# Batch 1's layer-norm statistics in one block, a pair earlier, and other work moved between engines in an attention, channel-mixer and gated-mixer kernel on one core

## What is computed

```
bits(q) == bits(k)                       # 6 hash bits by proj, bucket mask
attn = softmax(where(mask, q k^T / 8, -1e9)) v        -> x [2, 768, 512]
u    = x + real(fft(fft(x, tokens), features))
un   = (u - mean(u)) / sqrt(var(u) + 1e-6)
x2   = u + relu(un @ w_ch1) @ w_ch2                    # 512 -> 2048 -> 512
h    = gelu(x2 @ w_in);  U, v = split(h)
v_s  = w_sg @ (layernorm(v) * g_ln) + b_sg             # mixes tokens
out  = x2 + (U * v_s) @ w_out
```

## Time and profile before

| what | value |
|---|---|
| median of 3 runs | 735.77 us (735.25 to 736.75) |
| the profiled execution | 736.75 us, span of its instructions 734.9 us |
| PE busy | 716.1 us, 97% of the span, 3905 matmuls |
| DVE / ACT / POOL busy | 480.1 / 382.5 / 347.0 us |
| granted PE clock | 0.995 of full, mean |
| attention, transforms (about) | 0 to 260, 260 to 302.5 us |
| pairs 0 to 7, pairs 8 to 15 | 302.5 to 426.9, 426.9 to 558 us |
| gated mixer | from 563 us on |

### The profile page before, as it was taken

One profiled execution on the slowest core, in us unless ns is written; L12 is line 12 of the kernel. 1 busy time (PEld: TensorE's weight loads), 2 busy tenths in 40 slices (PEclk: granted clock), 3 DMA queues, 4 the chain that ended last, 5 costly groups with the idle time before them and its releaser, 6 DMA issues.

```text
span 734.9 us, 11758 instructions
## 1 busy us (share of the span) xinstructions
PE 716.1 (97%) x3905; PEld 590.5 (80%) x3905; DVE 480.1 (65%) x701; ACT 382.5 (52%) x708; POOL 347.0 (47%) x341
## 2 busy tenths in 40 slices
PE   8999999999999999999999999999999979999998
PEld 8857666666666899988888888999998868888886
DVE  6877787778786799876555677444434873247532
ACT  4867887888784635554444535445542553025300
POOL 4178878877887910224533261546542452004500
PEclk9999999999999999999999999999999989999999
DMA  4333323333243230121111212711003000010001
GB/s 97 69 73 67 77 60 71 73 67 70 60 101 115 69 113 1 42 74 58 58 58 58 70 46 101 243 58 58 29 1 144 0 1 0 29 58 1 0 15 72
DMA packets 71076, 45.20 MB, mean 62 GB/s; under 512 B 44996, under 2 KB 61560, under 8 KB 70520
## 3 DMA queue, kind: packets, MB, share of 16 engines
q1 hardware_dynamic: 70456, 41.19, 20.6%
q0 software_dynamic: 576, 3.43, 1.3%
HBM read 35.42 MB, written 3.15 MB: 52 GB/s over the span
## 4 chain that ended last, share of the span: by engine, by line
PE 86%; DVE 8%; ACT 2%; issue 2%; POOL 1%; DMA 1%; SPq 0%; POOLq 0%; ACTq 0%; DVEq 0%
PE PS L809 81%; DVE un L2007 2%; DVE mneg L1769 1%; PE PS L833 1%; PE PS L1096 1%; PE PS L1267 1%; PE PS L1313 1%; DMA ops<-mrow 1%; PE PS L1258 1%; PE PS L948 1%; DVE st L1995 0%; DVE W1L L2040 0%; DVE ops L1740 0%; DVE ops L1761 0%; DVE hL L2056 0%
## 5 line engine op out<-in xcount | busy, mean ns | idle before, releaser
L809 PE MATMUL PS<-ops 98*128 98x384 f32 (+1 forms) x576 | 134.8, 359 | 3.4 <-DMA ops<-mrow 1.1
L809 PEld LDWEIGHTS PS<-ops 98*128 98x128 f32 (+1 forms) x576 | 95.2, 189 | 44.1 <-ACT E L1380 19.6
L1769 DVE TENSOR_REDUCE mneg<-PS 128x1 f32<-128x768 f32 x96 | 91.5, 956 | 37.1 <-PE PS L809 36.5
L1380 ACT ACTIVATE E<-PS 128x384 f32<-128x384 f32 x192 | 83.5, 486 | 44.6 <-PE PS L809 43.8
L659 POOL TENSOR_TENSOR esum<-esum,E 128x768 f32<-128x768 f32 x56 | 102.5, 1830 | 2.9 <-ACT E L1380 0.3
L644 POOL TENSOR_TENSOR W2L<-W2R,W2H 128x1024 fp32r<-128x1024 f32 x16 | 38.5, 2407 | 114.7 <-ACT W2H L1364 114.7
L809 PE MATMUL PS<-BH,W1H 128*128 128x384 f32 x228 | 76.8, 337 | 2.8 <-DVE hL L2056 1.5
L2056 DVE SCALAR_TENSOR_TENSOR hL<-pre,hH 128x384 fp32r<-128x384 f32 x42 | 44.4, 1056 | 51.0 <-ACT hH L1625 51.0
L809 PE MATMUL PS<-BH,W1L 128*128 128x384 f32 x228 | 76.9, 337 | 0.0
L809 PE MATMUL PS<-BL,W1H 128*128 128x384 f32 x228 | 76.1, 334 | 0.0
L809 PE MATMUL PS<-W2H,hH 128*128 128x512 f32 x192 | 75.4, 393 | 0.0
(11 more groups left out here) (211 smaller groups left out, 1596.4 us busy)
## 6 DMA issues: line engine op xcount, KB each, us to landing
W1R<-in_moe_w_ch_dram SPq DMA_DIRECT2D x32, 256.0 KB, 3.1
W2R<-in_moe_w_ch_dram SPq DMA_DIRECT2D x32, 256.0 KB, 3.0
ops<-ops SPq DMA_DIRECT2D x30, 192.0 KB, 2.8
qk<-in_k_dram SPq DMA_DIRECT2D x32, 96.0 KB, 2.5
qk<-in_q_dram SPq DMA_DIRECT2D x32, 96.0 KB, 2.6
vn<-in_v_dram SPq DMA_DIRECT2D x32, 96.0 KB, 2.5
out_dram<-X SPq DMA_DIRECT2D x12, 256.0 KB, 2.0
WsgR<-in_moe_w_sg_dram SPq DMA_DIRECT2D x1, 2304.0 KB, 7.9
```

The source lines that it names most:

```text
L809: return pe.matmul(dst, lhs, rhs, start=start, stop=stop, **kw)
L1380: act.activation(A["E"][:, e_slot(t, 0, kt), half(a)], PS[:, ST_BANK + a, 0:HALF], ACT.Exp, scale=EXP_SCALE).then_inc(exp_done, 1)
L1769: dve.tensor_reduce(A["mneg"][:, s, j:j + 1], PS[:, bank:bank + 2, 0:HALF], AX.XY, ALU.max, negate=True).then_inc(max_done, 1)
```

## The change

1. SP no longer waits for the landing of the first `place_rows` before it goes on to the next loads.
2. ACT splits pair 1's weights (`weights_hi(1)`, three copies) behind the exponentials of the last head, in front of `fold_hi(1)`. Before, the three copies stood one by one between ACT's copies of groups 4 to 6 of batch 1's transform.
3. In the plain pairs DVE makes the first two token sums ahead of `hL` of C21, and the next pair's `W1L` between `hL` of C12 and the third token sum. Before, `W1L` came right after `hL` of C11 and the token sums were spread.
4. All six tiles of batch 1 get their statistics in DVE's pair 1, ahead of `hL` of C21; POOL's two `reciprocal_deviation(1, ...)` come ahead of `W2L` of pair 1. One tile is normalised and transposed in each of the pairs 1 to 6, not 2 to 7. PE's waits on the side bank follow.
5. The planes of batch 1's second token half (`un_hi`/`un_lo` 2 and 3) are made in pair 7 and no longer at the head of pair 8.
6. The first `second(8, ...)` of either block waits for both blocks of `channel_residual(0, ...)`: 18 on `x_upd`.
7. In the gated mixer `gate_lo` of tiles 0 to 3 of each batch moves from POOL to DVE, behind `mv` of two tiles later.

```
                 place_rows(fill, 1)
-                sp.wait_ge(rows_in, 32)
 
...
                     weight_sums(n + 1)
+                if n == 1:
+                    for block in range(2):
+                        reciprocal_deviation(1, block)
                 if n:
...
                     last_quarter(n)
-                if 1 <= n <= 2:
-                    reciprocal_deviation(1, n - 1)
                 if PAIRS + 3 <= n < PAIRS + 7:
...
 
-            def gate_lo(b, j):
-                pool.wait_ge(vh_done, b * T + j + 1)
-                pool.tensor_tensor(M2["VL"][:, j, :], M2["vr"][:, j % 3, :], rd(M2["VH"][:, j, :]), ALU.subtract).then_inc(vl_done, 1)
-
             for b in range(B):
...
                         scale_gate(N - 1, j - 1)
-                    if j >= 2:
-                        gate_lo(b, j - 2)
 
...
                         pe.wait_ge(pre_done, 2 * split_pairs(n))
-                    if 3 <= n < PAIRS:
-                        pe.wait_ge(ut_done, T + n - 2)
+                    if 2 <= n <= T + 1:
+                        pe.wait_ge(ut_done, T + n - 1)
                 elif step == P7:
...
                     if n:
-                        pe.wait_ge(ut_done, 2 * T)
+                        pe.wait_ge(pre_done, 2 * split_pairs(n))
                     else:
...
                     if b:
-                        pe.wait_ge(x_upd, NT + TH + TH * block)
+                        pe.wait_ge(x_upd, NT + T)
                     else:
...
                 product(n, P3)
-                if 2 <= n < PAIRS:
+                if n <= T:
                     pe.wait_ge(pre_done, 2 * split_pairs(n) + 2)
-                    un_transposes(T + n - 2, SIDE_BANK)
+                    un_transposes(T + n - 1, SIDE_BANK)
                 second(n - 1, C22)
...
 
-            def weights_hi(n, parts=range(3)):
+            def weights_hi(n):
                 if not plain(n):
...
                     act.wait_ge(w1_in[n % 2], 32 * (n // 2) + 32)
-                for i in parts:
-                    copy(M1["W1H"][:, n % 2, w1_parts(n)[i], :, :], w1_source(n, i)).then_inc(w1_hi, 1)
+                for i, rows in enumerate(w1_parts(n)):
+                    copy(M1["W1H"][:, n % 2, rows, :, :], w1_source(n, i)).then_inc(w1_hi, 1)
 
...
                     w2_upper(0)
+                if not t.looped and t.head(0) == HEADS - 1:
+                    weights_hi(1)
                 if not t.looped and t.head(0) == HEADS:
...
                         transformed_hi(b, p, pair)
-                        if b and 2 * p + pair < 3:
-                            weights_hi(1, (2 * p + pair,))
                 mirrored(b)
...
                 if plain(n):
-                    if n:
-                        un_hi(1, 2)
-                        un_hi(1, 3)
                     hidden_hi(n, C11)
...
                 w2_upper(n)
+                next_un(n, 2, P4)
                 hidden_hi(n, C21)
                 hidden_hi(n, C12)
-                if 2 <= n < PAIRS:
-                    un_copy(T + n - 2, SIDE_BANK)
+                if n <= T:
+                    un_copy(T + n - 1, SIDE_BANK)
+                next_un(n, 3, P3)
                 hidden_hi(n, C22)
...
                 if plain(n):
-                    if b:
-                        un_lo(b, 2)
-                        un_lo(b, 3)
                     hidden_lo(n, C11)
-                    weights_lo(n + 1)
-                    hidden_lo(n, C21)
                     token_sum(b, T1)
+                    token_sum(b, T2)
+                    hidden_lo(n, C21)
                     if b:
...
                     hidden_lo(n, C12)
-                    token_sum(b, T2)
-                    hidden_lo(n, C22)
+                    weights_lo(n + 1)
                     token_sum(b, T3)
+                    hidden_lo(n, C22)
                     un_lo(b, 4)
...
                 side_quarter(n, C21)
-                if 2 <= n < PAIRS:
-                    normalise(T + n - 2)
+                if n == 1:
+                    for c in range(T, NT):
+                        statistics(c)
+                    aggregate(1, 0)
+                    aggregate(1, 1)
+                if n <= T:
+                    normalise(T + n - 1)
+                next_un(n, 2)
                 hidden_lo(n, C21)
                 hidden_lo(n, C12)
+                next_un(n, 3)
                 hidden_lo(n, C22)
-                if n <= 2:
-                    for c in range(TH):
-                        statistics(T + TH * (n - 1) + c)
-                    aggregate(1, n - 1)
             channel_residual(1, 0, 4 * NP - 2)
...
                     dve.bn_aggr(M2["mv2"][:, j % 2, :], M2["st2"][:, j % 2, :]).then_inc(mv2_done, 1)
+                    if j >= 2:
+                        gate_lo(b, j - 2)
                     if b == 0:
...
                 centre_gate(b, T - 1)
-                dve.wait_ge(vl_done, b * T + T - 2)
                 gate_lo(b, T - 2)
```

More of the change, by code:

```diff
@@ L2099, in _ @@
                 if plain(n):
-                    if b:
-                        un_lo(b, 2)
-                        un_lo(b, 3)
                     hidden_lo(n, C11)
-                    weights_lo(n + 1)
+                    token_sum(b, T1)
+                    token_sum(b, T2)
                     hidden_lo(n, C21)
-                    token_sum(b, T1)
                     if b:
@@ L2109, in _ @@
                     hidden_lo(n, C12)
-                    token_sum(b, T2)
+                    weights_lo(n + 1)
+                    token_sum(b, T3)
                     hidden_lo(n, C22)
-                    token_sum(b, T3)
                     un_lo(b, 4)
```

## The result

The changed kernel takes 749.69 us (median of 4 runs, 748.81 to 750.48); the kernel before takes 736.26 beside it. The ratio is 1.0183, with a 95% interval of 1.0166 to 1.0202: slower by 13.4 us. The prediction was 748.0, with a range of 743.0 to 752.0.

What follows compares the result with a forecast made beforehand. PE is busy nearly the whole span, so time is lost only in its holes. Terms a to g sum to 9.35 us, 12.25 with one clock fall of 2.9, giving 748.0 against the median of 735.77; range 743.0 to 752.0.

Steps and rivals of the forecast that it cites:

- a: Scores of head 1: SP's next load can go 2.1 us earlier; -0.2 us, range -1.0 to +0.6.
- b: Second transform: three weight copies ahead of `fold_hi(1)` on ACT delay DVE, then PE; +1.85 us (0.9 to 1.9).
- c: Plain pair 0: P2 of pair 1 +0.15 us, P7 of pair 1 +0.5 through POOL and DVE alternating; +0.7 (0 to 1.2).
- d: Pair 1: PE's transposes wait for statistics, `mv`, `rstd`, `un`, a hole of 3.45 us; +3.85 us (3.3 to 4.8).
- e: Given back after d: shorter waits before transposes in pairs 2 and 3, -0.55 us; transposes gone from pair 7, -0.3.
- f: Pair 9: first `second` waits for block 1's residual too, POOL's sums alternating with DVE; hole 4.8 us, P7 +3.4 us.
- g: First mix of batch 0: `gate_lo` on DVE stands before the last tile's `WsgL`; +0.6 us (0.3 to 0.9).
- h: PE's clock at half behind f's hole, +2.9 us; none taken for d's hole, but a high chance left.
- The rival of two falls: The holes of d and f both lower PE's clock: 748.0 + 2.9 = 750.9 us; chance 0.35.

Runs made afterwards that it cites:

- the run with the filled holes: Changed kernel with half the filling matmuls of an earlier try, unread ident by ident, before pair 1's transposes and pair 9's first `second`: 745.93 us, ratio 1.0136.
- holding POOL back: Changed kernel with POOL's four weight sums for pair 10 held until DVE's last residual of pair 9 is done: 747.91 us, ratio 1.0157.
- the layer norm alone: Kernel before with only batch 1's layer norm moved as in the change, the last `un` splits a step later: 742.04 us, ratio 1.0076.
- `un` early: Kernel before with `normalise` in DVE's queue of pairs 2 to 7 ahead of `W1L` and of `pre` of C21: 732.44 us, ratio 0.9941.
- the other order: Kernel before with plain pairs reordered on DVE, T1 and T2 early and `W1L` ahead of `hL` of C12: 733.96 us, ratio 0.9959.
- the small moves: Kernel before with parts 1, 2 and 7 of the change (SP's wait, ACT's split of pair 1's weights, `VL` on DVE): 739.37 us, ratio 1.0045.

## Why the prediction was right, term by term

The waits are read where the clock is at full (the run with the filled holes), the clock from what is then left.

| term | predicted | measured |
|---|---|---|
| a, SP's wait | -0.2 | 0.0, give or take the 0.5 by which traces differ anyway |
| b, `weights_hi(1)` | +1.85 | +1.78 |
| c, plain pair 0 | +0.7 | +0.24 |
| d, statistics in pair 1 | +3.85 | +3.70 |
| e, given back | -0.85 | -0.61 |
| f, wait for 18 | +3.4 | +3.0 |
| g, `gate_lo` on DVE | +0.6 | +0.60 |
| sum of the waits | 9.35 | 8.7 |
| h, the clock | 2.9 | 3.0 in the profiled run, 4.7 left over in the median |

- **b, d, g** held by their own steps. Each was a queue without slack in front of a PE that waited for it already, or that stood just behind. In d the six statistics, `mv`, `rstd` and `un` took 330.63 + 0.55 - 325.53 = 5.65 us, and the hole in PE is 3.56 (3.38 from where the prediction counts, which had 3.45).
- **a** can't be told from nothing. At the end of attention's loop the six traces with this edit lie from 0.5 us early to 0.0 against that of before, and the seven others without it from 0.4 early to 0.3 late.
- **c** had P2's place right (0.16 us late, 0.15 predicted) and failed in its last step. DVE and POOL do alternate in pair 1 (1.49 for 0.95, twice), but the step to P7 of 0.5 didn't follow, because `pre` was still early enough. The collision was right, its victim was not on the path.
- **e**: pair 7's return was put at 0.3 and is 0.16, and pairs 2 and 3 gave 0.19 and 0.26, not 0.55 together.
- **f** had the mechanism and the hole (4.64 us, or 4.46 from where the prediction counts; 4.8 predicted), and a size 0.4 too high (3.08 at P7, of which 0.1 is gone again behind it). The alternation was taken as 1.6 us; holding POOL back shows 1.12. Without it P7 would start about 2.0 us late, an estimate from that run's trace (`second` 3.34 us late, less the 1.37 of waiting before P7 that goes), where the prediction had 1.7. But the wait alone, in DVE's old order, costs 2.8: the new order saves 0.8 of that and its alternation with POOL takes it back. The Trainium skill, "SBUF — State Buffer", section "SBUF: two separate sides", has the pair of ports that DVE and GpSimd share as an exclusive lock. The trace agrees in part. Alone, operations of these sizes follow each other every 0.87 us on DVE and every 0.70 on POOL, so taking strict turns would need 1.57 us for one of each; side by side they need about 1.4. That is near to turns, but it doesn't tell a lock from shared bandwidth.
- **h** was mis-sized in a way that cancelled against the rest. I gave one fall 2.9 us, from half of 5.80, and none to the hole of d. In the trace there are two falls, of 3.41 us each, and they cost 1.48 and 1.56 us (the shift over each hole, less the same in the run with filled holes). That two cheap falls come out as one dear one is luck. Against the median the waits are 0.65 too high and the clock 1.8 too low, which also cancels in part. The step that failed is the reason given for d, that no hole as short had been seen to lower the clock: none had been there to see. The trace of before has no hole between 1.7 us and the 3.98 before the mix (the prediction's "no hole as long as d's" is a slip, since that one is longer). The rival of two falls was right in its mechanism and, at 750.9, nearer to the 749.69 (1.2 us above) than the forecast (1.7 below); its waits and its price of a fall were both too high. "TensorE: Matmul & The Clock Gate" of the Trainium skill, section "What's actually happening", has idleness halve the clock; by it d's hole could count, and four traces out of four with an empty hole of 3.5 us in pair 1 show that it does.

The median lies 13.4 above before (12.2 to 14.9 by its interval) and the waits make 8.7, so about 4.7 us are left for the clock in an ordinary run. The runs' mean clocks fit that: 0.986 to 0.989 stand for 16 to 21 us at half clock, an estimate, where the profiled run has 13.65. Filling the two holes gives 3.3 to 3.8 back. The rest, 0.9 to 1.4, fits the fall behind b's hole, which five of the six traces with that hole show, at 1.4 to 1.5 us each; this wasn't tried by itself, by filling b's hole, and stays an inference.

The part that the prediction missed in the change as a whole is how much one line costs: the wait for both blocks is 4.7 us alone, about a third of the loss, and PE starts nothing earlier for it.

## What to carry to other kernels

When an in-order queue has no slack before the busiest engine's next wait, every instruction put into it costs nearly its full duration (1.78 of 1.89 us, and 0.60 of 0.66), and here nothing later gave it back; so look for the places where that queue itself waits for somebody, and put the extra work there (the new order of the plain pairs cost 0.5 us with `W1L` behind `hL` of C12 and gained 1.8 with it ahead). A wait should name exactly the data that is overwritten: a count that also took in the other block held PE for 2.8 us. Count a hole of PE twice, once for its length and once for the half clock that may follow it.

## What was not expected of the hardware

- The length of a hole doesn't decide alone whether the clock falls, or for how long. Behind the same hole of 3.97 us before the mix it stood at half for 6.83 us in four traces (before, the layer norm alone, the new order alone, `un` early), for 3.41 in one (the wait for 18 alone), and not at all in one (the other order). In the six traces with `gate_lo` on DVE that hole is 4.6 us, and the stretch was 6.83 in two (the changed kernel, the small moves) and 3.41 in four. A hole of 1.96 to 1.98 us lowered it in five traces of six; holes of 1.90 and 1.94 us before P7, and one of 1.86 before the mix in two traces, didn't. Where the same matmuls surround it, a hole's price for the clock is thus a spread, 0 to 2.7 us here, and not a number.
- It shows in the times, too: runs of the kernel before with a mean clock of 0.995 to 0.998 took 735.3 to 737.1 us, and the four at 0.993 took 738.6 to 739.2. With the hole before the mix cut to 1.86 us, all runs had 1.000 and lay within 0.6 us of each other.
- The clock can fall while PE still waits: in the run with the wait for 18 alone its mean over the hole is 0.74, so the low stretch had begun 2.2 us before PE resumed.
- A small weight sum of POOL (0.73 us alone) and a token operation of DVE (0.95 alone) each take 1.3 to 1.5 us when they run side by side in pair 9 (one of POOL's four took 0.73 there, beside DVE's `hL`, which reads PSUM); moved apart, DVE's are back at 0.95.
